# First block's tiles spread over more PSUM banks, low roundings behind all masks, queries scaled on VectorE, last store issued by ScalarE

## The reference, cut to what matters

```python
for t in range(S):                      # attention, float32
    state = alpha[:, :, t, :, None] * state + einsum('bhd,bhe->bhde', k[:, :, t], v[:, :, t])
    y[:, :, t] = einsum('bhd,bhde->bhe', q[:, :, t], state)
x = y.transpose(0, 2, 1, 3).reshape(3072, 384)
h = x @ w_in;  x = (h * clip(h + 3, 0, 6) / 6) @ w_out      # MLP 1: 384 -> 2048 -> 384
h = x @ w_in2; r = maximum(h, 0); result = (r * r) @ w_out2  # MLP 2
```

## Time and profile before

| what | value |
|---|---|
| median of 3 runs | 901.08 us (900.68 to 901.08) |
| the profiled execution's own time | 900.95 us |
| its span | 899.2 us |
| TensorE busy | 889.5 us, 99% of the span |
| VectorE, ScalarE, GpSimd busy | 317.0, 336.8, 311.2 us (35%, 37%, 35%) |
| chain that ended last | TensorE 97%, VectorE 1%, rest under 1% each |
| DMA queue 1 | 46.89 MB, 17.7% of 16 engines |
| first MLP matmul starts | 29.27 us |

### The profile page before, as it was taken

One profiled execution on the slowest core, in us unless ns is written; L12 is line 12 of the kernel. 1 busy time (PEld: TensorE's weight loads), 2 busy tenths in 40 slices (PEclk: granted clock), 3 DMA queues, 4 the chain that ended last, 5 costly groups with the idle time before them and its releaser, 6 DMA issues.

```text
span 899.2 us, 12769 instructions
## 1 busy us (share of the span) xinstructions
PE 889.5 (99%) x5052; PEld 736.2 (82%) x5052; DVE 317.0 (35%) x498; ACT 336.8 (37%) x600; POOL 311.2 (35%) x246
## 2 busy tenths in 40 slices
PE   8999999999999999999999999999999999999997
PEld 7788888888888888888888888888888888888886
DVE  7576445336425443452234431221121211211211
ACT  3744343333334333433344543332423332423332
POOL 2644243333424432433232333232323232323232
PEclk9999999999999999999999999999999999999999
DMA  9924222222320422220023200000000000000001
GB/s 289 323 59 108 57 55 56 56 55 55 96 61 9 107 57 55 55 56 10 6 100 106 71 1 0 36 1 1 36 0 1 36 1 1 35 1 1 36 0 37
DMA packets 22366, 47.73 MB, mean 53 GB/s; under 512 B 3617, under 2 KB 10017, under 8 KB 22305
## 3 DMA queue, kind: packets, MB, share of 16 engines
q1 hardware_dynamic: 22304, 46.89, 17.7%
HBM read 40.19 MB, written 4.72 MB: 50 GB/s over the span
## 4 chain that ended last, share of the span: by engine, by line
PE 97%; DVE 1%; DMA 0%; issue 0%; ACT 0%; DVEq 0%
PE h_ps L750 44%; PE o_ps L763 44%; PE att_ps L670 3%; PE att_ps L705 2%; PE att_ps L708 2%; PE att_ps L681 1%; PE att_ps L724 1%; DVE x_mid L508 1%; DMA x_mid<-att_in 0%; DVE x_mid L513 0%; PE o_ps L691 0%; PE h_ps L657 0%; PE att_ps L691 0%; DVE h_gate L539 0%; DVE masked_t L539 0%
## 5 line engine op out<-in xcount | busy, mean ns | idle before, releaser
L365 POOL TENSOR_TENSOR g_parts<-h_act,g_parts 128x512 fp32r<-128x512 f32 x192 | 252.6, 1316 | 563.5 <-ACT g_parts L431 563.5
L763 PE MATMUL o_ps<-g_parts,w_out_hi 128*128 128x512 f32 x1152 | 326.9, 389 | 0.0
L750 PE MATMUL h_ps<-x_parts,w_in_hi 128*128 128x512 f32 x1152 | 297.6, 394 | 0.2 <-ACT x_parts L406 0.2
L763 PEld LDWEIGHTS o_ps<-g_parts,w_out_hi 128*128 128x128 f32 x1152 | 216.3, 188 | 44.9
L750 PEld LDWEIGHTS h_ps<-x_parts,w_in_hi 128*128 128x128 f32 x1152 | 213.0, 188 | 45.3 <-issue 0.7
L431 ACT ACTIVATE g_parts<-h_act 128x512 fp32r<-128x512 f32 x192 | 121.3, 632 | 290.1 <-PE o_ps L763 240.2
L569 DVE SCALAR_TENSOR_TENSOR h_act<-h_ps,h_gate 128x512 f32<-128x512 f32 x96 | 66.4, 691 | 290.5 <-ACT h_gate L426 290.5
L763 PE MATMUL o_ps<-g_parts,w_out_lo 128*128 128x512 f32 x576 | 165.6, 389 | 0.0
L750 PE MATMUL h_ps<-x_parts,w_in_lo 128*128 128x512 f32 x576 | 161.8, 389 | 0.0
L566 DVE SCALAR_TENSOR_TENSOR h_act<-h_gate,h_ps 128x512 f32<-128x512 f32 x96 | 65.6, 683 | 183.8 <-ACT h_gate L423 183.8
L750 PEld LDWEIGHTS h_ps<-x_parts,w_in_lo 128*128 128x128 f32 x576 | 108.1, 188 | 22.7
(11 more groups left out here) (89 smaller groups left out, 404.6 us busy)
## 6 DMA issues: line engine op xcount, KB each, us to landing
inputs<-att_in SPq DMA_DIRECT2D x20, 451.5 KB, 4.3
inputs<-att_in SPq DMA_DIRECT2D x20, 448.0 KB, 5.6
w_in_raw<-w_in SPq DMA_DIRECT2D x8, 768.0 KB, 10.7
w_out_raw<-w_out SPq DMA_DIRECT2D x8, 768.0 KB, 11.2
result<-inputs SPq DMA_DIRECT2D x18, 256.0 KB, 2.3
inputs<-v_in SPq DMA_DIRECT2D x20, 192.0 KB, 5.7
x_parts<-tails SPq DMA_DIRECT2D x120, 16.0 KB, 3.0
x_mid<-att_in SPq DMA_DIRECT2D x4, 451.5 KB, 7.9
```

Of the source, the lines that this page charges most:

```text
L365: nc.gpsimd.tensor_tensor(g_parts[:, g % 2, 1, :], h_act[:, g % 2, :], g_parts[:, g % 2, 0, :].bitcast(F32), ALU.subtract).then_inc(g_lo, 1)
L750: last = nc.tensor.matmul(h_ps[g % 2][:, :], w[:, m, cols], x_parts[:, n % 2, part, m, :], start=m == 0 and i == 0, stop=m == KT - 1 and i ...
L763: return nc.tensor.matmul(o_ps[m][:, :], w[:, f, m * P:(m + 1) * P], g_parts[:, g % 2, part, :], start=f == 0 and w is w_out_hi and part = ...
```

## The change

Five edits. Line numbers of the new code differ from those of before; names are the same.

1. `banks`: tile 2's scores and y use `h_ps[0]` and `h_ps[1]`, its keys `att_ps[2]`; tile 3 uses `att_ps[1]` and `o_ps[1]` for scores and `o_ps[2]` for keys. The wait of `score` on the low rounding of tile t - 2 is gone for the first block; tile 3 waits for the masks of tile 1. The low roundings of all four tiles move behind the last mask on VectorE, and `hidden(0)`, which writes `h_ps[0]`, waits for three of them.
2. Queries of tiles 1 and 2 are scaled by VectorE; GpSimd scales only their keys.
3. Tile 0's alpha comes in two transfers of 112x516 values, and the first scan waits for the first of them.
4. Order: the values of tiles 2 and 3 are loaded ahead of the first two weight groups; on ScalarE the first two `split_w` move to behind the range check of tile 2; on TensorE `add_up(2)` comes ahead of `score(3)`, `attend_first(2)` behind it. `WARM_UP` becomes (16, 8, 3, 5).
5. ScalarE issues the last store itself.

```diff
-WARM_UP = (16, 8, 5, 8)
+WARM_UP = (16, 8, 3, 5)
...
         def banks(t):
-            return o_ps if t in (1, 3) else att_ps
+            first = {1: o_ps, 2: (h_ps[0], h_ps[1], att_ps[2]), 3: (att_ps[1], o_ps[1], o_ps[2])}
+            return first.get(t, att_ps)
...
-                sp.dma_start(slot(t)[0:ROWS, 0:ALPHA_W], att_in[t, :, 0:ALPHA_W]).then_inc(a_loaded[slot_of(t)], 16)
+                begin = 0
+                if t == 0:
+                    begin = PAIRS * REV
+                    sp.dma_start(from_end(t), att_in[t, :, 0:begin]).then_inc(first_loaded, 16)
+                sp.dma_start(slot(t)[0:ROWS, begin:ALPHA_W], att_in[t, :, begin:ALPHA_W]).then_inc(a_loaded[slot_of(t)], 16)
...
+            load_values(2)
+            load_values(3)
             load_w(0)
-            load_values(2)
             load_w(1)
-            load_values(3)
...
                 nc.gpsimd.tensor_tensor(keys(t), keys(t), revs(from_end(t))[:, :, 0:TILE], ALU.mult).then_inc(k_scaled, 1)
+                if t < BATCH:
+                    return
...
                 if g >= FT and f == LAG - 1:
                     evacuate(n - 1)
+                    if n == 2 * NBLK:
+                        act.wait_ge(o_free[KT - 1], 2 * NBLK + 1)
+                        act.dma_start(out[(KT - 1) * P:, (NBLK - 1) * BLK:], out_stage[:, KT - 1, :]).then_inc(out_stored, 16)
...
             make_decays(0)
-            scale(0)
+            scale_keys(0)
+            scale_queries(0)
             make_decays(1)
             mask(0)
+            scale_queries(1)
             make_decays(2)
-            x_low(0)
             mask(1)
+            scale_queries(2)
             make_decays(3)
-            x_low(1)
-            scale(3)
+            scale_keys(3)
+            scale_queries(3)
             mask(2)
             mask(3)
-            x_low(2)
-            x_low(3)
+            for t in range(BATCH):
+                x_low(t)
...
                         pe.wait_ge(x_hi, hi_parts(BATCH * (n + 1) - 1))
+                        if n == 0:
+                            pe.wait_ge(x_lo, hi_parts(BATCH - 2))
```

More of the change, by code:

```diff
@@ L179, in banks @@
         def banks(t):
-            return o_ps if t in (1, 3) else att_ps
+            first = {1: o_ps, 2: (h_ps[0], h_ps[1], att_ps[2]), 3: (att_ps[1], o_ps[1], o_ps[2])}
+            return first.get(t, att_ps)
         def masked_of(t):
             return h_gate[:, :, :].rearrange("p a (b c) -> p a b c", b=PAIRS) if t in (1, 3) else masked_t[:, :, :, :]
-        def bank_user_before(t):
-            return t - 1 if t > 4 else t - 2
         def x_cols(t, part):
@@ L206, in chunked_program @@
         act_warm = sem("act_warm")
+        first_loaded = sem("first_loaded")
         a_loaded = [sem(f"a_loaded{i}") for i in range(BATCH + 2)]
@@ L340, in _ @@
             for n in range(NBLK):
-                for m in range(KT):
+                for m in range(KT if n < NBLK - 1 else KT - 1):
                     sp.wait_ge(o_free[m], NBLK + n + 2)
@@ L464, in _ @@
             x_high(1)
-            split_w(0)
             first_state(1)
@@ L468, in _ @@
             check_ranges(2)
+            split_w(0)
+            first_state(2)
+            copy_keys(3)
             split_w(1)
             x_high(2)
-            copy_keys(3)
-            first_state(2)
             x_high(3)
@@ L505, in make_decays @@
                 nc.vector.memset(seed_cols, 1.0).then_inc(seeded, 1)
-                wait_loaded(dve, a_loaded, t)
+                if t == 0:
+                    dve.wait_ge(first_loaded, 16)
+                else:
+                    wait_loaded(dve, a_loaded, t)
                 dve.wait_ge(seeded, 2 * t + 1)
@@ L514, in make_decays, with scale_keys @@
                                              ALU.max).then_inc(to_token_made, 1)
-            def scale(t):
+            def scale_keys(t):
                 wait_loaded(dve, kq_loaded, t)
@@ L519, in scale, with scale_queries @@
                 nc.vector.tensor_tensor(keys(t), keys(t), revs(from_end(t))[:, :, 0:TILE], ALU.mult).then_inc(k_scaled, 1)
+            def scale_queries(t):
+                wait_loaded(dve, kq_loaded, t)
                 dve.wait_ge(to_token_made, t + 1)
-                past(dve, q_scaled, t)
                 nc.vector.tensor_tensor(queries(t), queries(t), revs(to_token(t))[:, :, 0:TILE], ALU.mult).then_inc(q_scaled, 1)
@@ L656, in warm_up @@
                 for _ in range(WARM_UP[i]):
-                    nc.tensor.matmul(h_ps[0][:, 0:P], ident[:, :], ident[:, :], start=True, stop=True)
+                    nc.tensor.matmul((att_ps[1] if i == 3 else h_ps[0])[:, 0:P], ident[:, :], ident[:, :], start=True, stop=True)
             def score(t):
                 bank_even, bank_odd, _ = banks(t)
-                before = bank_user_before(t)
                 pe.wait_ge(k_scaled, t + 1)
                 pe.wait_ge(q_scaled, t + 1)
-                if before >= 0:
-                    pe.wait_ge(x_lo, hi_parts(before))
-                    pe.wait_ge(masked, 2 * (before + 1))
+                if t == BATCH - 1:
+                    pe.wait_ge(masked, 2 * (t - 1))
+                if t >= BATCH:
+                    pe.wait_ge(x_lo, hi_parts(t - 1))
+                    pe.wait_ge(masked, 2 * t)
                 for j in range(PAIRS):
@@ L676, in turn_keys @@
                 bank_k = banks(t)[2]
-                before = bank_user_before(t)
-                if before >= 0:
-                    pe.wait_ge(state_made, 2 * (before + 1))
+                if t >= 2:
+                    pe.wait_ge(state_made, 2 * (t if t >= BATCH else t - 1))
                 for j in range(PAIRS):
@@ L714, in add_up @@
                 pe.wait_ge(k_back_copied, t + 1)
+                wait_loaded(pe, v_loaded, t)
                 for j in range(PAIRS):
@@ L800, in _ @@
             turn_keys(2)
+            pe.wait_ge(masked, 2)
             warm_up(3)
+            add_up(2)
             score(3)
+            turn_keys(3)
             attend_first(2)
-            add_up(2)
-            turn_keys(3)
             attend_first(3)
```

## The result

| | before | changed |
|---|---|---|
| median | 900.98 us (8 runs, 900.50 to 902.20) | 903.70 us (8 runs, 902.31 to 905.65) |
| ratio | 1 | 1.0031, 95% interval 1.0021 to 1.0042 |
| profiled execution: own time, span | 900.95, 899.2 | 903.47, 901.7 |
| last matmul's end to the span's end | 4.66 | 4.65 |
| first MLP matmul | 29.27 | 31.27 |

A forecast was written before the change was run, and what follows sets the result against it. TensorE bounds 97% of the chain, so time can only be won before the first MLP matmul and after the last. Head 0.35 plus tail 0.6 is 0.95 off the median 901.08: 900.1 us, range 898.7 to 901.1.

The forecast's parts named there:

- VectorE's part: Head, up to tile 1's masks: four changes sum to 1.5 us, so the masks end near 16.9 instead of 18.33.
- the long scan: VectorE's scan at 12.95 took 2.24 us, others 1.23; without GpSimd's query scaling beside it, 1.0 comes back.
- the 0.7: Gain in us taken for VectorE's first scan, which waits for only half of the first load.
- TensorE's part: Head, from tile 1's masks on: y of tile 3 ends at 26.2 to 26.6 instead of 28.70.
- my 27: Start of the first MLP matmul if nothing but TensorE's work held it: near 27, over 2 us sooner.
- The weights: w_in lands near 23.9, w_out at 26.3; ScalarE's roundings follow, first MLP matmul 28.9 instead of 29.27: head gives 0.35.
- The clock: Rival, chance 0.06: idling over 2 us ahead of the MLP drops TensorE's clock for 5 us, +2.5: 902.6.
- The tail: After the last matmul: ScalarE issues the third store at 895.2 without waiting for SyncE's queue, 0.6 us sooner.
- my lower bound of 0.1: Least gain at the end of the kernel: ScalarE's store takes 3.5 us like the second store, landing at 898.7.
- The sequencer's time, 0.83: End of the kernel: the third store's wait for SyncE's queue, the most that issuing from ScalarE could save.
- my two terms: Head up to the first MLP matmul, 0.35 (-0.3 to 0.9), and tail after the last, 0.6 (0.1 to 1.0).

The follow-up runs named there:

- keys: The kernel before with tile 0's keys and queries loaded in two transfers instead of one, nothing else changed: 902.62 us, ratio 1.0027.
- The tenth place in the queue: The kernel before with tile 3's keys and queries in two transfers, the tenth and eleventh of the queue: 900.73 us, ratio 0.9999.
- the other queue: The changed kernel with both high roundings ahead of the w_out split and the first transfer's second half issued by ScalarE: 899.04 us, ratio 0.9981.
- the old order: The changed kernel with w_in, values 2, w_out, values 3 loaded in the order of before: 903.50 us, ratio 1.0021.

## Why the prediction was wrong

*VectorE's part.* Right in its terms: first scan 0.81 sooner (0.7 said), the long scan back to 1.23, tile 1's masks done at 17.40 in the change (16.9 said). Wrong in one thing: it let the 0.7 run through to the masks, while the next tile's alpha, late by the split, stopped VectorE for 0.73.

*TensorE's part.* Right in its length. y of tile 3 was said to end at 26.2 to 26.6. It ended at 27.3 in the change, where the 0.7 was lost and tile 3's keys were late, and at 27.2 with the transfer whole and the roundings first, which has no 0.7 to gain: that kernel's 27.77 for the first MLP matmul is my 27 with the 0.7 put back.

*The weights.* This is the step that failed. "The four transfers hold the same bytes in either order, so the one that is last now, `w_out`, lands where the last values did, at 26.3" took the rate of the queue from the kernel before, and the sentence on the split, "the second half is needed one scan and a reciprocal later and bounds nothing", weighed only who waits for that half, not what its transfer does to those behind it. I counted every byte and not the transfers. With the first transfer whole, `w_in` came to ScalarE at 24.23 and `w_out` at 27.08: 0.3 and 0.8 off my figures, and the first MLP matmul at 29.64 where I had said 28.9. With it split, they came at 25.54 and 28.71. The 0.8 that is left in that profile is within what the landing varies by: with the roundings first as well, the same order landed `w_out` at 25.9, on the other side of my 26.3. The mechanism, the order on ScalarE that lets `w_out` hold back the roundings, was right, and moving it was worth 1.3 us (900.69 to 899.36).

*The clock.* The rival that I gave 0.06 did happen, but only behind the late weights: 2.5 us of idle time where I had reckoned with about 2. Its price was also off: the lower level lasted from about 32.8 to 36.2, not 5 us, it cost 1.5 instead of 2.5, and two thirds of that came out of waits that were there anyway. The Trainium skill, TensorE: Matmul & The Clock Gate, section What's actually happening, has an idle stretch bring the throttled level back; the trace agrees, with 0.50 granted from 33 to 36. One reading of the rival has no such support: the profile's granted clock stands at 1.00 from 2 to 9 us of the kernel before, so the lower level at the start, and the 5 us to leave it, rest on the lengths of the warm-up matmuls alone.

*The tail.* 0.6 was said; eight profiles of nine give 0.5 against the 4.66 of before, and the one of the change gives nothing, because ScalarE's store took 3.6 us to land and not 3.0 to 3.2. That is below even my lower bound of 0.1. The sequencer's time, 0.83, was not reached in any. Alone, the moved store gave 0.2 in the median, which is not told from nothing.

*The range.* Its upper edge, 901.1, held no case in which the queue as a whole is slower. It even lay below what my two terms give at their worst ends, -0.3 and 0.1 off 901.08, which is 901.3. The one case it should have had was a price for the added transfer, whose only row was the rate of the queue without it.

## What to carry to other kernels

A transfer split to let its first half come sooner is one more transfer in a queue that is full behind it; read the rate of the whole stretch, not only the arrival of the half. Ahead of a move, ask what each in-order engine has queued behind the wait that becomes longer: here two roundings that TensorE needed stood behind a weight that nobody needed for six microseconds. Measure each edit of a bundle alone: of these five one cost 3 us, and with it mended and one order changed the rest gives 1.5 to 1.8. What the PSUM banks and VectorE's scaling of the queries give, each by itself, was not measured.

## What the runs showed that I had not expected

One transfer more near the start of SyncE's queue lowers the rate of everything behind it for 15 us and more, with the DMA engines busy throughout. Between 3 and 24 us the profiles without it moved 327 (before), 342 (store alone), 320 (first transfer whole), 333 and 339 GB/s (whole, roundings first, either order). The profiles with it moved 312, 249, 275, 274 (the change and its variants), 258 (split alone), 284 (keys) and 267 (by partitions). The tenth place in the queue (340) and the other queue (334) are harmless.

The size of the effect varies from profile to profile, and the change's own profile is the mildest case. Its 312 against 320 is 0.17 MB by 24 us, about 0.5 us by my estimate from these rates, where `w_out` landed 1.6 later (28.7 against 27.1). Tile 3's keys landed there 3.4 us behind the transfer ahead of them (18.1 to 21.5), with the first transfer whole 1.7 (17.3 to 18.9). So in that execution the mean rate is not the whole of it.

What in the queue does it stays open. The full rows of the split by partitions and the unchanged bytes rule out both as the explanation, and no run here looks inside a DMA engine's queue. Every added transfer was made by cutting another in two, so an added transfer beside whole ones is untried, and so is the split with its second half issued later. The Trainium skill, DMA: Bandwidth & Descriptors, section Issuing engines are not separate DMA queues, lets issuing from two engines save only the sequencer's time; for the first transfer the measurement differs, since with the roundings first the same half transfer costs 2.6 us on one queue (901.98 against 899.36 for the whole one) and nothing on the other (899.04).

TensorE's clock did not fall in the idle stretch but 1.5 us into the work behind it. Nor does the length of the stretch settle it: 1.78 us of idle time left it at 2.4 GHz in the profile with the whole transfer, and behind 1.77 us, in the profile with the old order, it fell to 1.2 GHz at about 27.6, 0.8 us into the work. Three of the eleven executions with the whole transfer show a lower mean clock and take 1.5 to 2 us more; how long TensorE idled in them is not known. A price for an idle stretch of about 2 us is thus at best a chance times a price.
